# An attention and MLP kernel on one core: the head pair's splits, the low-rank constants and the first loads are scheduled in another order

## The reference

```
q_rot, k_rot = rotate(q), rotate(k)                  # rotary: x*cos + swapped(x)*sin
attn = softmax(q_rot @ k_rot^T / sqrt(64))
x = (attn @ v), heads side by side                   # (4, 576, 512)
u = x + (x^T @ U @ V)^T                              # U: 576x32, V: 32x576, over the sequence
out = u + relu(u @ w_ch1) @ w_ch2
```

## Time and profile before

| | us |
|---|---|
| median of 3 runs | 767.85 |
| lowest, highest | 767.82, 769.2 |
| the profiled execution | 767.85 |
| its span in the profile | 766.0 |

### The profile page before, as it was taken

One profiled execution on the slowest core, in us unless ns is written; L12 is line 12 of the kernel. 1 busy time (PEld: TensorE's weight loads), 2 busy tenths in 40 slices (PEclk: granted clock), 3 DMA queues, 4 the chain that ended last, 5 costly groups with the idle time before them and its releaser, 6 DMA issues.

```text
span 766.0 us, 12193 instructions
## 1 busy us (share of the span) xinstructions
PE 709.4 (93%) x4252; PEld 638.2 (83%) x4252; DVE 402.5 (53%) x660; ACT 437.9 (57%) x942; POOL 464.4 (61%) x338
## 2 busy tenths in 40 slices
PE   1899887799999999999999999999999799999998
PEld 1788885699998878989999988789998578999996
DVE  3799876655556775444454466665554651112111
ACT  1788865666766665565555565666665233333331
POOL 2788946384849664674865966639333135665653
PEclk9999989999999999999999999999999999999999
DMA  6987683628383628439366284473532054445352
GB/s 215 252 217 198 153 234 112 201 72 227 100 264 92 178 82 235 165 110 264 102 190 201 81 210 138 140 200 97 143 118 76 28 170 152 153 138 165 125 169 78
DMA packets 74700, 119.59 MB, mean 156 GB/s; under 512 B 27152, under 2 KB 27280, under 8 KB 72848
## 3 DMA queue, kind: packets, MB, share of 16 engines
q1 hardware_dynamic: 73760, 117.27, 52.1%
q10 hardware_dynamic: 880, 1.54, 0.6%
HBM read 81.04 MB, written 9.44 MB: 118 GB/s over the span
## 4 chain that ended last, share of the span: by engine, by line
PE 69%; DVE 8%; POOL 7%; ACT 7%; issue 5%; DMA 4%; SPq 0%; POOLq 0%; ACTq 0%; DVEq 0%
PE ps L991 24%; PE ps L1007 22%; PE ps L901 7%; PE ps L915 7%; PE ps L935 5%; POOL raw L503 2%; DMA stack<-raw 2%; ACT prob L635 2%; DVE negmax L769 2%; POOL raw L504 1%; PE ps L928 1%; DVE utl L845 1%; PE ps L973 1%; POOL w2l L566 1%; ACT uth L672 1%
## 5 line engine op out<-in xcount | busy, mean ns | idle before, releaser
L560 POOL TENSOR_TENSOR w1l<-w1u,w1h 128x512 fp32r<-128x512 f32 x96 | 123.9, 1291 | 236.9 <-ACT w1h L679 236.9
L769 DVE TENSOR_REDUCE negmax<-ps 128x1 f32<-128x576 f32 (+1 forms) x160 | 120.3, 752 | 62.5 <-PE ps L901 59.5
L854 DVE SCALAR_TENSOR_TENSOR htl<-ps,hth 128x384 fp32r<-128x384 f32 x96 | 53.5, 557 | 186.3 <-ACT hth L690 186.2
L901 PE MATMUL ps<-stack 128*128 128x288 f32 (+1 forms) x640 | 119.1, 309 | 31.3 <-DMA stack<-raw 19.5
L646 ACT ACTIVATE pth<-ps 128x512 fp32r<-128x512 f32 x162 | 91.1, 566 | 89.2 <-PE ps L935 87.4
L635 ACT ACTIVATE prob<-ps,negmax 128x576 f32<-128x576 f32 (+1 forms) x160 | 117.9, 737 | 32.9 <-DVE negmax L769 30.0
L991 PE MATMUL ps<-uth,w1h 128*128 128x384 f32 x384 | 132.1, 344 | 2.2 <-DVE utl L845 2.2
L901 PEld LDWEIGHTS ps<-stack 128*128 128x128 f32 (+1 forms) x640 | 95.8, 182 | 45.0 <-issue 20.6
L991 PE MATMUL ps<-uth,w1l 128*128 128x384 f32 x384 | 129.4, 337 | 0.0
L991 PE MATMUL ps<-utl,w1h 128*128 128x384 f32 x384 | 129.2, 336 | 0.0
L690 ACT ACTIVATE hth<-ps 128x384 fp32r<-128x384 f32 x96 | 47.1, 490 | 140.0 <-PE ps L991 139.8
(11 more groups left out here) (69 smaller groups left out, 1086.0 us busy)
## 6 DMA issues: line engine op xcount, KB each, us to landing
w1u<-in_w SPq DMA_DIRECT2D x96, 256.0 KB, 2.7
w2u<-in_w SPq DMA_DIRECT2D x96, 256.0 KB, 2.7
stack<-raw SPq DMA_DIRECT2D x64, 288.0 KB, 4.4
raw<-in_qk SPq DMA_DIRECT2D x14, 1152.0 KB, 5.7
stack<-raw SPq DMA_DIRECT2D x62, 144.0 KB, 3.9
v2u<-in_v SPq DMA_DIRECT2D x16, 320.0 KB, 4.0
res<-scratch_u SPq DMA_DIRECT2D x18, 256.0 KB, 4.0
out<-res SPq DMA_DIRECT2D x18, 256.0 KB, 2.4
```

The source lines that it names most:

```text
L560: nc.gpsimd.tensor_tensor(w1l[:, at], w1u[:, at], w1h[:, at], ALU.subtract).then_inc(w1_lo, 1)
L769: nc.vector.tensor_reduce(negmax[0:WT[t], t:t + 1], scores_of(n, WT[t]), AX.XY, ALU.max, negate=True).then_inc(maxed, 1)
L901: mm = nc.tensor.matmul(ps[0:WT[t], at + c * BANK:at + c * BANK + CH], stack[:, g % HEADS_STACKED, 0, P * t:P * t + WT[t]], stack[:, g % H ...
```

## The change

Five things are scheduled otherwise; what is computed stays the same.

1. Pair 0 on DVE: each `first_products` becomes two instructions of 576 elements, and `first_lo(1)` (the remainder of k) comes after the products of q.
2. First loads: SP no longer waits for head 0's copies; `stack_q(0, 1)` goes to ACT's queue, right behind `stack_q(0, 0)`; on SP the load of pair 1's k comes at once, then `load_v(0)`, then `stack_k(0, 1)`.
3. Pairs 1 to 5 on POOL: `split_lo` of q and k leave `rope` and stand in slots 2 and 4 of the pair, as those of the other pairs do.
4. Low-rank constants: loaded in slot 0 behind `load(2)`; rounded by ACT in slot 5 (`NT` is 5); remainders by DVE in slot 6; nothing of it on POOL.
5. ACT rounds v of pair 0 in slot 1 and not in slot 4.

```diff
-FIRST_V = 4
-LOW_RANK = 28
+FIRST_V = 1
@@ SP, ahead of the slots
             sp.wait_ge(lo_split[0], 1)
-            sp.wait_ge(stacked[0], STACKED)
-            stack_q(sp, 0, 1)
             sp.dma_start(raw[:, 1, :, 1], qk[1][:, :, 1]).then_inc(first_loaded, 16)
+            load_v(0)
             stack_k(sp, 0, 1)
-            load_v(0)
             load_v(1)
@@ SP, slots
-                if n == STACK:
-                    sp.dma_start(uraw, u4).then_inc(mix_loaded, 16)
-                    sp.dma_start(vmraw, v4).then_inc(mix_loaded, 16)
                 if s == LOAD and r + 3 < NPAIRS:
                     load(r + 3)
                 if n == 0:
                     load(2)
+                    sp.dma_start(uraw, u4).then_inc(mix_loaded, 16)
+                    sp.dma_start(vmraw, v4).then_inc(mix_loaded, 16)
@@ POOL
                     nc.gpsimd.tensor_copy(both[:, 1].bitcast(F32R), both[:, 0]).then_inc(qk_hi[which], 1)
-                    split_lo(r, which)
-                if s == SPLIT_Q + 1 and r not in POOL_ROUNDS:
+                if s == SPLIT_Q + 1:
                     split_lo(r, 0)
-                if s == SPLIT_K + 1 and r not in POOL_ROUNDS:
+                if s == SPLIT_K + 1:
                     split_lo(r, 1)
-            def split_low_rank():
...
-                if n == LOW_RANK:
-                    split_low_rank()
@@ ACT
             act.wait_ge(lo_split[0], 1)
-            stack_q(act, 0, 0)
+            for j in range(2):
+                stack_q(act, 0, j)
...
+                if n == NT:
+                    act.wait_ge(mix_loaded, 32)
+                    nc.scalar.activation(us[:, :, :], uraw, ACT.Copy).then_inc(mix_consts, 1)
+                    nc.scalar.activation(vs[:, :], vmraw, ACT.Copy).then_inc(mix_consts, 1)
@@ DVE
-                both = raw[:, 0, :, which]
-                nc.vector.tensor_tensor(both, both, tables[:, :, which], ALU.mult).then_inc(first_rope, 1)
+                x, xs = raw[:, 0, 0, which], raw[:, 0, 1, which]
+                nc.vector.tensor_tensor(x, x, cos_t[:, which], ALU.mult).then_inc(first_rope, 1)
+                nc.vector.tensor_tensor(xs, xs, sin_t[:, which], ALU.mult).then_inc(first_rope, 1)
...
             first_sum(1)
-            first_lo(1)
             dve.wait_ge(q_tables, 32)
             dve.wait_ge(raw_loaded[0], 16)
             first_products(0)
+            first_lo(1)
             first_sum(0)
             first_lo(0)
...
+                if n == NT + 1:
+                    dve.wait_ge(mix_consts, 2)
+                    second = slice(R, 2 * R)
+                    nc.vector.tensor_tensor(us[:, :, 3 * R:P], uraw[:, :, 3 * R:P],
+                                            us[:, :, 3 * R:P], ALU.subtract).then_inc(mix_consts, 1)
+                    nc.vector.tensor_tensor(vs[second, :], vmraw[second, :], vs[second, :],
+                                            ALU.subtract).then_inc(mix_consts, 1)
```

More of the change, by code:

```diff
@@ L739, in first_products @@
             def first_products(which):
-                both = raw[:, 0, :, which]
-                nc.vector.tensor_tensor(both, both, tables[:, :, which], ALU.mult).then_inc(first_rope, 1)
+                x, xs = raw[:, 0, 0, which], raw[:, 0, 1, which]
+                nc.vector.tensor_tensor(x, x, cos_t[:, which], ALU.mult).then_inc(first_rope, 1)
+                nc.vector.tensor_tensor(xs, xs, sin_t[:, which], ALU.mult).then_inc(first_rope, 1)
             def first_sum(which):
                 x, xs = raw[:, 0, 0, which], raw[:, 0, 1, which]
-                dve.wait_ge(first_rope, 1 if which else 2)
+                dve.wait_ge(first_rope, 2 if which else 4)
                 nc.vector.tensor_tensor(x, x, xs, ALU.add).then_inc(roped[which], 1)
```

## The result

| | before | changed |
|---|---|---|
| first comparison, median (lowest to highest) | 769.48 us (767.47 to 773.37, 8 runs) | 775.14 us (771.99 to 776.78, 8 runs) |
| second comparison | 769.64 us (29 runs) | 776.64 us (6 runs) |
| profiled execution | 767.85 us | 771.76 us, span 770.0 us |

The ratio is 1.0058 with a 95% interval of 1.003 to 1.0086 in the first comparison, 1.0082 (1.0064 to 1.0101) in the second; the medians alone would give 1.0074 and 1.0091. The direction was forecast; the median of 775.14 lies above the range, which ended at 773.5. Both kernels spread over 5 to 6 us, more than the three runs shown ahead of the prediction had told, and the profiled execution of before (767.85 us) is one of its fastest.

The account below looks back on a forecast made before the run. PE bounds the kernel (69% of the chain), so early delays move the end: 767.85 us + 1.65 (+3.3 for the constants' wait, -1.67 at slot 40) + 1.7 for the clock = 771.2 us; range 766.9 to 773.5.

Parts of the forecast that it names:

- slots 8 to 10 (slack, DVE, clock): Slots 8 to 10: PE's present 0.15 us wait absorbs some delay, DVE's part is hidden, lower clock costs 1.7 us.
- That the constants decide, and how: Slot 5: ACT waits 2.6 us for the low-rank constants, rounds them in 1.3 us; slot 8's scores come 3.5 us later.
- When the constants land: Behind load(2), issued once pair 0's heads are stacked at 24.5 us: constants land at 32.3 us, bounds 29.4 and 33.5.
- low bound: Earliest landing of the constants: all bytes at 365 GB/s, pair 0 stacked at 21.8 us, constants there at 29.4 us.
- Head 0 later by 0.8 us, head 1 not: First copies: q copies share DMA engines with a load, head 0 starts near 17.9 us; head 1 at 26.4, as now.
- The equal share: Head 0's q copies and a 0.59 MB load share the DMA engines equally: copies take 3.0 us, +1.5 us.
- The rule of the Trainium skill: First copies: DMAs started by several engines share 16 DMA engines, so a second queue gives no bandwidth; head 0 +1.5 us.
- DVE's remainders lie beside PE: Slot 6: remainders of 0.4 and 0.75 us on DVE are covered by PE's work; 1 us if that cover were gone.
- POOL's new order costs nothing: Pairs 1 to 5 on POOL: later q remainder costs nothing; up to 1.2 us a pair if q copies fall behind k copies.
- The stop at slot 40: Slot 40: without POOL's 3.5 us low-rank split, pair 4's copies land earlier; gain 1.67 us, bounds 0 and 1.67.
- The clock: Slots 8 and 9: after PE idles some 4 us, clock falls to 1.2 GHz, losing 1.7 us, at most 3.4.
- No change from slot 50 to the end, and a base of 767.85 us: Distance from slot 50 to the end stays the same; the sum starts from the profiled execution, 767.85 us.

Follow-up runs that it names:

- second trace: The changed kernel unaltered, run and traced a second time; this execution took 776.78 us, and the median of its comparison was 776.64 us.
- part 4 alone: Kernel before, with only the low-rank constants loaded behind load(2), rounded by ACT in slot 5, remainders on DVE in slot 6: 775.5 us, ratio 1.0060.
- the constants ahead: Changed kernel with both low-rank constant loads moved ahead of the wait of load(2), behind v of pair 1: 773.29 us, ratio 1.0038 to the kernel before.
- POOL held: Changed kernel with constants loaded ahead of load(2), and POOL waiting before pair 2's rotary until DVE made both remainders: 770.87 us, ratio 1.0014 to before.
- the split in slot 45: Kernel before, with the low-rank split left on POOL but moved from slot 28 to slot 45: 769.3 us, ratio 0.9987.
- the remainders in slot 45: Changed kernel with constants loaded ahead of load(2), and both remainders made by POOL in slot 45, not DVE: 772.04 us, ratio 1.0036 to before.

## Why the prediction was right and wrong

The mechanism held; the size was too small. The terms of the sum against the two traces, in us:

| stretch | forecast | first trace | second trace |
|---|---|---|---|
| up to slot 8 | +3.5 | +4.4 | +5.2 |
| slots 8 to 10 (slack, DVE, clock) | -0.15 and +1.7 | +0.3 | +1.6 |
| slots 10 to 40 | -1.7 | -1.5 | -1.7 |
| slots 40 to 50 | 0 | -1.1 | -1.1 |
| slot 50 to the end | 0 | +1.8 | +4.9 |
| sum | +3.4 | +3.9 | +8.9 |

- **That the constants decide, and how.** Right. ACT waits for a DMA in slot 5, PE idles in front of slot 8, part 4 alone gives 1.0060, and without it nothing is left (1.0001).
- **When the constants land.** Mis-sized. The copies of head 1 were to be complete at 24.5 us, at 25.7 at the latest; `load(2)` was issued at 25.91 and 26.43. The constants were forecast for 32.3 us and came at 33.3 and 34.1; that is the +0.9 and +1.7 of the first line. The list of transfers left out v of pair 1, issued at 18.90 and landed 7.9 us later in the first trace; by the prediction's own rate of loads it is up to 0.9 us, an estimate. (Its low bound, 21.8 + 6.1 + 1.7, is 29.6 and not 29.4.) ACT waited 0.94 and 1.73 us and not 2 to 3, because ACT came there at 32.4 us in both traces and not at 29.7, behind a late head 1.
- **Head 0 later by 0.8 us, head 1 not.** Mis-sized, and the path was wrong: +3.7 and +2.5 us. The q copies took 6.6 us from issue to scores in the first trace and 7.5 in the second, against 3.8 before; in the first they were also issued 0.9 us later (14.20 and not 13.33). Head 0's slots took 8.0 us and head 1 had waited 0.75, so the slack was 1.2 us and the other 2.5 went on to head 1. The equal share that I took as the upper bound (+1.5) left out v of pair 0 and the copies of head 1, which were in the queues with the load. The rule of the Trainium skill quoted for this step ("DMA: Bandwidth & Descriptors", section "Issuing engines are not separate DMA queues"), with its +1.5 us, had the right sign and was still too small. The late start hides behind the wait for the constants: part 4 alone, with head 0 at 16.58 us, is no faster.
- **DVE's remainders lie beside PE.** This step of part 4 failed. They were sized at 1.15 us with bounds of 0.6 and 2.1; they took 2.2 us, up to 3.8 with the constants ahead, because they wait for POOL's instruction. In the first trace that put slot 9 0.75 us behind PE, of which 0.3 was left at slot 10; beside a longer POOL instruction, in the kernel with the constants ahead, it cost more (8.4 us from slot 8 to slot 10 against 4.3 with POOL held, the clock included).
- **POOL's new order costs nothing.** True in the whole change, false alone (1.0038).
- **The stop at slot 40.** Right: -1.48 and -1.7 us in the traces of the changed kernel, -1.68 with the split in slot 45.
- **The clock.** Right for the second trace and the kernel with part 4 alone, wrong for the first, where it stayed at 1.00 behind slot 8. It differs from execution to execution of one kernel. The mean over the executions with a record of it is 0.990 for the changed kernel (16) and 0.992 for before in each of the three comparisons of experiments; 0.002 of 770 us is about 1.5 us of work at full speed, an estimate.
- **No change from slot 50 to the end, and a base of 767.85 us.** This is the step that put the median outside the range. The distance was named as a sign of being wrong if it changed, and it was 1.8 and 4.9 us longer. Two traces of the same changed kernel differ by 3.1 us in it, and the trace from which the sum started had 645.2, the second shortest of fourteen; its 767.85 us lie 1.6 us below the median of eight (769.48) and further below those of the later comparisons. Whether the change has a part in the rest stays open: the seven traces of kernels with the constants' rounding in slot 5 have 645.8 to 651.0 us, the seven others 645.0 to 647.5. Against its own base the range ended at +0.74%; the first comparison measured +0.58% by the ratio, inside, and +0.74% by the medians, just at the end; the second +0.82% by the ratio, outside.
- **Size.** That the sum at slot 10 (+5.0) lies near the first trace (+4.7) is luck in part: 0.9 us of late constants and 0.4 us behind slot 8 stand against 1.7 us of clock that this execution did not lose.

## What to carry to other kernels

When small jobs move from an engine with slack to two engines in the critical loop, price three things: what the load has to wait behind, the job itself, and what its operands share with the engine that was freed. A DVE instruction with both operands in SBUF is not free beside a busy POOL; put it where POOL rests, or hold POOL. And a wait that seems idle in the first microseconds may guard the one transfer that everything waits for: without it head 0 started 3.7 us later, and the transfers queued earlier were complete no earlier. Last, take the base of a sum from several executions: here one trace was 1.6 us faster than the median, in a stretch that nobody touched.

## What was not expected of the hardware

DVE and POOL: 0.33 us grew to 1.91, 0.75 to 1.90. It goes both ways: POOL's rounding took 1.08 us when it was issued while DVE's remainder ran (36.34 above) and 0.66 elsewhere.

The same stop of 3.19 us at slot 46 had the clock fall in the trace of before, and not in the first trace of the changed kernel. The same stop of 1.64 us ahead of slot 8 was followed by 3.4 us at 1.2 GHz in the trace with the remainders in slot 45, and by none in the one with POOL held. The length of the stop alone does not tell.

Another source of spread is far from the change. In the second trace of the changed kernel PE waits 2.31 us at slot 109 for a chain that begins with a weight load of 8.3 us (issue at 358.15), in the first it does not:

```profile
369.82 0.47 PE L1000 MATMUL ps<-w2h,hth 128*128 128x512 f32 x1 [2.31 <-DVE htl L840]
ACT w1h L660 <- DMA w1u<-in_w: 3.6, 1, 3.6
```
